# A convolution and two MLPs on one core: TensorE's instruction stream as one loop in place of seven passes written out

## The chip, the core and the metric

The kernel runs on one core of one Trainium2 chip. The core has five engines, each with an instruction queue of its own: PE (TensorE, matmuls), DVE (VectorE), ACT (ScalarE), POOL (GpSimd) and SP (SyncE, which here issues nearly all the DMAs). They meet only through semaphores. The metric is the time of one execution on the device, in microseconds (us). Before the change it is 1183.47 us, the median of 3 runs (1183.36 to 1183.52).

## The reference

The input x has 2 x 4096 rows of 192 numbers. Three things are done to it in turn: a causal filter over time with 7 softmax-weighted taps per head, and two MLPs from 192 to 2048 and back to 192.

```python
w = softmax(weight, axis=-1)                     # 8 heads, 7 taps
attn = sum over k of w[head, k] * x_pad[s + k]   # causal, zeros ahead of row 0
x1 = attn.reshape(8192, 192)

h = x1 @ moe_w_in                                # 192 -> 2048
x2 = np.maximum(0.01 * h, h) @ moe_w_out         # leaky, back to 192

h = x2 @ moe2_w_in
g = np.where(h >= 1, h, np.where(h <= -1, 0.0, (h + 1) ** 2 / 4))
out = g @ moe2_w_out
```

All of it is float32 in the reference.

## The kernel before

**Tiles and jobs.** The 8,192 rows are cut into 16 tiles of 512. Each tile is a leaky job (first MLP) and later a smooth job (second MLP), 32 jobs in all. A job takes the 2,048 hidden units in 16 chunks of 128. For a chunk, PE makes the hidden block (192 rows of weights against 512 columns of the tile, in high and low parts of the numbers, so that the product is as exact as float32), ACT and DVE apply the activation and split the result into a high part `g_hi` and a low part `g_lo`, and PE multiplies these by the second weights into two accumulators, `acc_edge` and `acc_main`.

**Matmuls in pairs.** Nearly every matmul uses 64 of the 128 rows of the array. `top_first` and `top_second` use the upper half, `bottom_first` and `bottom_second` the lower, and the code writes them in turn, so that one of either half runs at a time. One step of `two_chunks` writes 38 matmuls: 18 that open two chunks and finish the pair six chunks back (lines 338 to 348 and 430 to 442), then 20 in `second_half` (lines 401 to 414 and 360 to 374). A job has 8 such steps, 304 matmuls.

**Order.** Each engine's program is written by hand. The first two jobs fill the pipeline. Then come 7 passes (`PASSES`) of four jobs each, `loop_jobs(j)`: smooth, leaky, smooth, leaky. Then two last smooth jobs.
Of the kernel before, what the change touches and what calls it, by code (L numbers as in the profile page):

```python
# [34 lines left out]
def is_number(v, *numbers):  # L35

    return type(v) is int and v in numbers
# [7 lines left out]
def bass_conv_mlp_mlp(nc, x, weight, moe_w_in, moe_w_out, moe2_w_in, moe2_w_out, out):  # L45
# [24 lines left out]
    with ExitStack() as ctx:  # L70
# [112 lines left out]
        def leaky_job(n, a, t, b, prev, load=None, finish=None, at=4):  # L183
            return dict(n=n, a=a, at=at, layer=LEAKY, t=t, b=b, prev=prev, load=load, finish=finish)

        def smooth_job(n, a, t, b, prev, finish=None):
            return dict(n=n, a=a, layer=SMOOTH, t=t, b=b, prev=prev, load=None, finish=finish)

        first_jobs = [
            leaky_job(0, 0, 0, EVEN, None, load=(1, ODD, 0), finish=(1, ODD), at=1),  # L190
            leaky_job(1, 1, 1, ODD, (LEAKY, 0, EVEN), load=(2, EVEN, 1)),
        ]
        PASSES = (TILES - 2) // 2

        def loop_jobs(j):

            return [
                smooth_job(4 * j + 2, 0, 2 * j, EVEN, (LEAKY, 2 * j + 1, ODD), finish=(2 * j + 2, EVEN)),
                leaky_job(4 * j + 3, 1, 2 * j + 2, EVEN, (SMOOTH, 2 * j, EVEN),
                          load=(2 * j + 3, ODD, j + 1)),  # L200
                smooth_job(4 * j + 4, 0, 2 * j + 1, ODD, (LEAKY, 2 * j + 2, EVEN), finish=(2 * j + 3, ODD)),
                leaky_job(4 * j + 5, 1, 2 * j + 3, ODD, (SMOOTH, 2 * j + 1, ODD),
                          load=(2 * j + 4, EVEN, j + 2)),
            ]

        last_jobs = [
            smooth_job(2 * TILES - 2, 0, TILES - 2, EVEN, (LEAKY, TILES - 1, ODD)),
            smooth_job(2 * TILES - 1, 1, TILES - 1, ODD, (SMOOTH, TILES - 2, EVEN)),
        ]
        JOBS = 2 * TILES  # L210

        def all_jobs(engine, run):
            for job in first_jobs:
                run(job)
            with engine.Fori(0, PASSES) as j:
                for job in loop_jobs(j):
                    run(job)
            for job in last_jobs:
                run(job)
# [13 lines left out]
        def _(sp):  # L233
# [18 lines left out]
            def load_weights(piece):  # L252
                l, q = piece // PIECES, piece % PIECES
                s, _, _, rows, _ = piece_parts(piece)
                loaded = stage_loaded[piece % AHEAD]
                w = w_in_dram[l][:, q * PW:(q + 1) * PW]
                sp.dma_start(s[:, 0:PW], w[0:P]).then_inc(loaded, 16)
                for r in (0, EDGE):
                    sp.dma_start(s[r:r + EDGE, PW:2 * PW], w[P:D]).then_inc(loaded, 16)
                sp.dma_start(rows, w_out_dram[l][:, q * PC:(q + 1) * PC, :]).then_inc(loaded, 16)  # L260
# [60 lines left out]
        def _(pe):  # L321
# [155 lines left out]
            def opening(job):  # L477

                for i in range(5):
                    top_first(job, 0, i)
                for i in range(2):
                    top_first(job, 1, i)
                for i in range(2):
                    top_first(job, 1, i + 2)
                    bottom_first(job, 0, i)
                for i in range(2):
                    top_first(job, 2, i)
                    bottom_first(job, 0, i + 2)  # L490
                for i in range(3):
                    top_first(job, 2, i + 2)
                    bottom_first(job, 1, i)
                for i in range(2):
                    top_first(job, 3, i)
                    bottom_first(job, 1, i + 3)
                for i in range(2):
                    top_first(job, 3, i + 2)
                    bottom_first(job, 2, i)
                for i in range(2):  # L500
                    top_first(job, 4, i)
                    bottom_first(job, 2, i + 2)
                for i in range(3):
                    top_first(job, 4, i + 2)
                    bottom_first(job, 3, i)
                for i in range(2):
                    top_first(job, 5, i)
                    bottom_first(job, 3, i + 3)
                for i in range(2):
                    top_first(job, 5, i + 2)  # L510
                second_half(job, 4)

            def two_chunks(job, c):

                for i in range(5):
                    top_first(job, c, i)
                    bottom_second(job, c - 6, i)
                for i in range(4):  # L520
                    top_first(job, c + 1, i)
                    bottom_second(job, c - 6, i + 5)
                second_half(job, c)

            def run(job):
                opens = is_number(job["n"], 0)
                if opens:
                    opening(job)
                for c in range(6 if opens else 0, CHUNKS, 2):
                    two_chunks(job, c)  # L530
                if is_number(job["n"], 1):
                    pe.wait_ge(stage_used, 2 * PIECES)
# [8 lines left out]
            pe.wait_ge(warm_ready, 1)  # L541
            for _ in range(WARM):
                nc.tensor.matmul(acc_main[1][:], g[0][:, 0:P], g[0][:], start=True, stop=True)
            for job in first_jobs:
                run(job)
            for j in range(PASSES):
                for job in loop_jobs(j):
                    run(job)
            for job in last_jobs:
                run(job)  # L550
            for i in range(10):
                bottom_second(last_jobs[-1], CHUNKS - 6, i)
            for c in range(CHUNKS - 4, CHUNKS):
# [3 lines left out]
        def _(act):  # L557
# [46 lines left out]
            def top_smooth(prev):  # L604

                _, t, b = prev
                act.wait_ge(edge_step, 2 * t + 1)
                nc.scalar.copy(op_top[SMOOTH][b][EDGE:P, :], edge_sum[:]).then_inc(op2_top_ready, 1)
# [58 lines left out]
        def _(dve):  # L667
# [99 lines left out]
            def between_main(prev, a):  # L767

                _, t, b = prev
                dve.wait_ge(op2_hi_ready, t + 1)  # L770
                nc.vector.tensor_tensor(op_lo[SMOOTH][b][:], acc_main[a][:],
                                        op_hi[SMOOTH][b][:].bitcast(F32), ALU.subtract).then_inc(acc_taken, 1)
# [131 lines left out]
```

## Time and profile before

| | |
|---|---|
| Median of 3 runs | 1183.47 us |
| The profiled execution | 1183.36 us |
| Its span, first to last instruction | 1181.6 us |
| PE matmuls busy | 1155.8 us, 98% of the span |
| PE weight loads busy (they overlap the matmuls) | 924.5 us, 78% |
| DVE busy | 920.8 us, 78% |
| ACT busy | 793.2 us, 67% |
| POOL busy | 61.1 us, 5% |
| Granted TensorE clock, mean | 0.992 of full speed |

The profile is of one execution, and its times are read against that execution's 1183.36 us. Of PE, the profile has two kinds of rows: matmuls and weight loads as the array ran them, and on PE's queue (written PEldq) the semaphore, register and branch instructions as the queue executed them. The queue runs ahead of the array. Rows with ACTq, DVEq and SPq are of the other engines' queues. "q8 instruction" and "q14 instruction" are DMA queues that bring instructions, not data. In a strip of 40 slices, each digit is the busy share of a fortieth of the stretch in tenths, and serves here to place a packet in time. The clock is given as a share of 2.4 GHz: 1.00 is that, 0.50 is 1.2 GHz.

### The profile page before, as it was taken

The page shows a single profiled execution, that of the slowest core. Times are in us where ns is not written, and L with a number is a line of the kernel's source. Part 1 is how long each engine was busy: PE and PEld are TensorE (multiplying, and loading weights), DVE is VectorE, ACT ScalarE, POOL GpSimd, SP SyncE. Part 2 cuts the span into 40 slices and gives each one's busy share as a digit, 9 for nine tenths or more (in the row PEclk, how much of TensorE's full clock was granted, in tenths as well). Part 3 has the DMA queues.
Part 4 walks back from the last instruction along what each step waited for, and adds up shares of the span by engine and source line. Part 5 has one row for each costly group of instructions (what it writes and reads, how often), then busy time and mean ns, then how long its engine had stood idle before and what let it go on. Part 6 is the DMA issues. An engine that isn't in the chain of part 4 may idle for free.

```text
span 1181.6 us, 25758 instructions
## 1 busy us (share of the span) xinstructions
PE 1155.8 (98%) x9726; PEld 924.5 (78%) x9726; DVE 920.8 (78%) x1525; ACT 793.2 (67%) x1457; POOL 61.1 (5%) x73
## 2 busy tenths in 40 slices
PE   6889999999999999999999999999999999999998
PEld 3567888888888888888888888888888888888886
DVE  6988787777888778787777788777887777878665
ACT  3566757667585775757667585675857667586685
POOL 4762000000000000000000000000000000000000
PEclk8989999999999999999999999999999999999999
DMA  4330010010101001010010101001010010100001
GB/s 120 90 86 10 1 28 1 14 17 1 28 1 28 3 1 28 1 28 3 12 17 1 29 2 28 1 2 29 1 28 1 12 19 1 28 1 15 1 1 27
DMA packets 114468, 22.18 MB, mean 19 GB/s; under 512 B 106128, under 2 KB 114320, under 8 KB 114320
## 3 DMA queue, kind: packets, MB, share of 16 engines
q1 hardware_dynamic: 114304, 20.34, 9.3%
q8 instruction: 77, 1.26, 0.5%
q14 instruction: 71, 0.58, 0.2%
q10 hardware_dynamic: 16, 0.00, 0.0%
HBM read 14.02 MB, written 6.29 MB: 17 GB/s over the span
## 4 chain that ended last, share of the span: by engine, by line
PE 92%; DVE 5%; ACT 1%; issue 1%; SPq 0%; DMA 0%; DVEq 0%; ACTq 0%
PE hidden L348 14%; PE hidden L340 10%; PE acc_edge L404 10%; PE hidden L342 9%; PE acc_edge L401 9%; PE hidden L344 9%; PE acc_main L412 9%; PE acc_main L414 9%; PE acc_main L410 9%; DVE conv_main L691 1%; DVE g L748 1%; DVE conv_edge L703 1%; DVE g_lo L759 0%; ACT pre L577 0%; ACT g_hi L596 0%
## 5 line engine op out<-in xcount | busy, mean ns | idle before, releaser
L596 ACT CAST g_hi<-g 128x512 fp32r<-128x512 f32 x512 | 300.4, 619 | 300.2 <-PE acc_main L442 247.4
L759 DVE TENSOR_TENSOR g_lo<-g,g_hi 128x512 fp32r<-128x512 f32 x512 | 335.7, 690 | 120.7 <-ACT g_hi L596 116.0
L348 PE MATMUL hidden<-op_edge,w_edge 64*128 64x512 f32 x768 | 262.2, 395 | 1.6 <-DVE op_edge L736 1.6
L753 DVE SCALAR_TENSOR_TENSOR g<-hidden,pre 128x512 f32<-128x512 f32 x256 | 176.7, 690 | 105.6 <-ACT pre L584 102.6
L340 PE MATMUL hidden<-op_hi,w_main 64*128 64x512 f32 x512 | 203.5, 398 | 13.1 <-DVE op_lo L716 5.7
L360 PE MATMUL hidden<-op_hi,w_main 64*128 64x512 f32 x512 | 202.4, 395 | 0.0
L404 PE MATMUL acc_edge<-g_lo,w_out 64*128 64x512 f32 x508 | 200.8, 395 | 1.5 <-DVE g_lo L759 1.5
L342 PE MATMUL hidden<-op_lo,w_main 64*128 64x512 f32 x512 | 202.1, 395 | 0.0
L364 PE MATMUL hidden<-op_hi,w_main 64*128 64x512 f32 x512 | 202.0, 395 | 0.0
L344 PE MATMUL hidden<-op_hi,w_main 64*128 64x512 f32 x512 | 201.9, 394 | 0.0
L362 PE MATMUL hidden<-op_lo,w_main 64*128 64x512 f32 x512 | 201.4, 393 | 0.0
L367 PE MATMUL hidden<-op_edge,w_edge 64*128 64x512 f32 x512 | 201.2, 393 | 0.0
L430 PE MATMUL acc_edge<-g_hi,w_out 64*128 64x512 f32 x508 | 200.5, 395 | 0.0
L440 PE MATMUL acc_main<-g_hi,w_out 64*128 64x512 f32 x508 | 200.4, 394 | 0.0
L432 PE MATMUL acc_edge<-g_lo,w_out 64*128 64x512 f32 x508 | 199.9, 393 | 0.0
L442 PE MATMUL acc_main<-g_lo,w_out 64*128 64x512 f32 x508 | 199.8, 393 | 0.0
L401 PE MATMUL acc_edge<-g_hi,w_out 64*128 64x512 f32 x508 | 199.8, 393 | 0.0
L438 PE MATMUL acc_main<-g_hi,w_out 64*128 64x512 f32 x508 | 199.8, 393 | 0.0
L412 PE MATMUL acc_main<-g_hi,w_out 64*128 64x512 f32 x508 | 199.4, 392 | 0.0
L410 PE MATMUL acc_main<-g_hi,w_out 64*128 64x512 f32 x508 | 199.4, 392 | 0.0
L414 PE MATMUL acc_main<-g_lo,w_out 64*128 64x512 f32 x508 | 199.4, 392 | 0.0
L748 DVE SCALAR_TENSOR_TENSOR g<-pre 128x512 f32<-128x512 f32 x256 | 181.7, 715 | 22.5 <-ACT pre L577 22.3
(92 smaller groups left out, 2805.4 us busy)
## 6 DMA issues: line engine op xcount, KB each, us to landing
x_in<-in_x_dram SPq DMA_DIRECT2D x68, 64.0 KB, 2.3
out_dram<-y_main SPq DMA_DIRECT2D x64, 64.0 KB, 1.8
stage<-in_moe_w_out_dram SPq DMA_DIRECT2D x16, 192.0 KB, 2.7
x_in_edge<-in_x_dram SPq DMA_DIRECT2D x68, 32.0 KB, 2.0
stage<-in_moe_w_in_dram SPq DMA_DIRECT2D x16, 128.0 KB, 2.4
stage<-in_moe_w_in_dram SPq DMA_DIRECT2D x32, 64.0 KB, 2.4
out_dram<-y_edge SPq DMA_DIRECT2D x32, 64.0 KB, 1.8
taps_raw<-in_weight_dram ACTq DMA_DIRECT2D x1, 0.2 KB
```

Source lines behind the costliest of these rows:

```text
L340: nc.tensor.matmul(h[:], w_main[l][top, 0, cols], op_hi[l][b][top, :], start=True, stop=False)
L342: nc.tensor.matmul(h[:], w_main[l][top, 0, cols], op_lo[l][b][top, :], start=False, stop=False)
L344: nc.tensor.matmul(h[:], w_main[l][top, 1, cols], op_hi[l][b][top, :], start=False, stop=False)
L348: done = nc.tensor.matmul(h[:], w_edge[l][top, i - 3, cols], op_edge[l][b][top, :], start=False, stop=False)
L360: nc.tensor.matmul(h[:], w_main[l][bottom, 0, cols], op_hi[l][b][bottom, :], start=False, stop=False)
L401: nc.tensor.matmul(edge[:], w[:, P:2 * P], hi, start=k == 0, stop=False)
L404: done = nc.tensor.matmul(edge[:], w[:, P:2 * P], lo, start=False, stop=False)
L410: nc.tensor.matmul(main[:], w[:, 0:P], hi, start=k == 0, stop=False)
L412: nc.tensor.matmul(main[:], w[:, 2 * P:], hi, start=False, stop=False)
L414: done = nc.tensor.matmul(main[:], w[:, 0:P], lo, start=False, stop=False)
L596: nc.scalar.copy(g_hi[c % SLOTS][:], g[c % SLOTS][:]).then_inc(g_hi_ready, 1)
L759: nc.vector.tensor_tensor(g_lo[c % SLOTS][:], g[c % SLOTS][:], g_hi[c % SLOTS][:].bitcast(F32), ALU.subtract).then_inc(g_lo_ready, 1)
```

## The change

PE's program now calls `all_jobs` as ACT's and DVE's do. The helper is not changed:

```python
        def all_jobs(engine, run):
            for job in first_jobs:
                run(job)
            with engine.Fori(0, PASSES) as j:
                for job in loop_jobs(j):
                    run(job)
            for job in last_jobs:
                run(job)
```

```diff
@@ -541,13 +541,7 @@
             pe.wait_ge(warm_ready, 1)
             for _ in range(WARM):
                 nc.tensor.matmul(acc_main[1][:], g[0][:, 0:P], g[0][:], start=True, stop=True)
-            for job in first_jobs:
-                run(job)
-            for j in range(PASSES):
-                for job in loop_jobs(j):
-                    run(job)
-            for job in last_jobs:
-                run(job)
+            all_jobs(pe, run)
             for i in range(10):
                 bottom_second(last_jobs[-1], CHUNKS - 6, i)
```

In the built program PE's stream had 9,717 matmuls and 292 semaphore instructions in one piece. Now it has 567 matmuls ahead of the loop, 1,216 in its body and 638 behind it. The body also has 129 register operations, 16 fused register operations (shown as ISA), 30 semaphore instructions and the compare-and-branch; for the same four jobs the program before has 36 semaphore instructions and nothing else beside its matmuls. The order of the matmuls is the same. No other engine's program changes.

On PE, at the seam of two passes, the program before goes from the last matmuls of one leaky job straight to the first ones of the next smooth job:

```order
L412 MATMUL acc_main<-g_hi,w_out 128x512
L367 MATMUL hidden<-op_edge,w_edge 128x512
L414 MATMUL acc_main<-g_lo,w_out 128x512
L374 MATMUL hidden<-op_top,w_edge 128x512
L340 MATMUL hidden<-op_hi,w_main 128x512 [waits g_ready,op2_ready]
L430 MATMUL acc_edge<-g_hi,w_out 128x512 [waits edge_top_added]
L342 MATMUL hidden<-op_lo,w_main 128x512
```

On PE at the end of the loop's body the same matmuls are now followed by the loop's own instructions, L215, which is the line of `Fori`:

```order
L412 MATMUL acc_main<-g_hi,w_out 128x512
L367 MATMUL hidden<-op_edge,w_edge 128x512
L414 MATMUL acc_main<-g_lo,w_out 128x512
L374 MATMUL hidden<-op_top,w_edge 128x512
L215 REGISTER_ALU
L215 COMPARE_AND_BRANCH
```

The branch goes back to the head of the body, whose first rows on PE are these:

```order
L215 ISA
L339 ISA [waits op2_ready]
L340 MATMUL hidden<-op_hi,w_main 128x512 [waits g_ready]
L429 ISA
L430 MATMUL acc_edge<-g_hi,w_out 128x512 [waits edge_top_added]
L342 MATMUL hidden<-op_lo,w_main 128x512
L432 MATMUL acc_edge<-g_lo,w_out 128x512
L344 MATMUL hidden<-op_hi,w_main 128x512
L430 MATMUL acc_edge<-g_hi,w_out 128x512
```

The matmuls stand as before. Three fused register operations have come between them, and the wait on `op2_ready` has moved from a semaphore instruction to one of these.

## Rows read from the trace of the kernel before

**Rows 1.** The page: busy time with share and count; shares of the chain.

```profile
PE 1155.8 (98%) x9726; PEld 924.5 (78%) x9726; DVE 920.8 (78%) x1525; ACT 793.2 (67%) x1457; POOL 61.1 (5%) x73
...
PE 92%; DVE 5%; ACT 1%; issue 1%; SPq 0%; DMA 0%; DVEq 0%; ACTq 0%
```

**Rows 2.** Windows of one pass: stretch, busy us and count by engine, clock, DMA.

```profile
core 0: us, PE busy (x) PEld busy (x) DVE busy (x) ACT busy (x) POOL busy (x), PEclk, DMA share, GB/s
248.40:390.20 141.80, 141.80 (x1220) 114.44 (x1218) 111.43 (x188) 97.01 (x176) 0.00 (x0) 1.00 0.08 13
```

**Rows 3.** PE's timeline over two seams: start, us, instruction.

```profile
246.19 0.39 PE L414 MATMUL acc_main<-g_lo,w_out 64*128 64x512 f32 x1
...
246.43 0.40 PE L340 MATMUL hidden<-op_hi,w_main 64*128 64x512 f32 x1
...
388.29 0.40 PE L340 MATMUL hidden<-op_hi,w_main 64*128 64x512 f32 x1
```

**Rows 4.** The page, instruction queues: packets, MB, share of 16 engines.

```profile
q8 instruction: 77, 1.26, 0.5%
q14 instruction: 71, 0.58, 0.2%
```

**Rows 5.** L215 on ACT's queue, 246 to 256 us: count, ns, first and last start.

```profile
L215 ACTq ALU_OP  x1: 35/35/35, 249.0 to 249.0; - x1
L215 ACTq COMPARE_BRANCH  x1: 54/54/54, 249.0 to 249.0; - x1
L215 ACTq FUSED_REGOPS  x1: 68/68/68, 251.5 to 251.5; - x1
```

**Rows 6.** L215 on DVE's queue, the same stretch.

```profile
L215 DVEq COMPARE_BRANCH  x1: 63/63/63, 250.2 to 250.2; - x1
L215 DVEq FUSED_REGOPS  x1: 85/85/85, 253.2 to 253.2; - x1
```

**Rows 7.** L282 on SP's queue, 230 to 240 us.

```profile
L282 SPq COMPARE_BRANCH  x1: 59/59/59, 235.6 to 235.6; - x1
L282 SPq FUSED_REGOPS  x1: 50/50/50, 235.8 to 235.8; - x1
```

**Rows 8.** DMA in 40 slices of 249:251, then of 252.5:254.5, with instruction queues.

```profile
DMA  0000000000000000000400000000000000000000
...
q14 instruction: 1, 0.01, 1.2%
...
DMA  0000000000090000000000000600000000000000
...
q8 instruction: 1, 0.02, 3.7%
```

**Rows 9.** L400 on PE's queue, 414 to 416 us, and the matmul behind it.

```profile
L400 PEldq EVENT_SEMAPHORE  x1: 51/51/51, 415.2 to 415.2; - x1
...
416.99 0.39 PE L401 MATMUL acc_edge<-g_hi,w_out 64*128 64x512 f32 x1
```

**Rows 10.** L339 and L400 on PE's queue, 422 to 424.5 us.

```profile
L339 PEldq EVENT_SEMAPHORE  x1: 51/51/51, 422.6 to 422.6; - x1
...
L400 PEldq EVENT_SEMAPHORE  x1: 51/51/51, 424.1 to 424.1; - x1
```

**Rows 11.** L339 on PE's queue, 103 to 104 us, and its matmul.

```profile
L339 PEldq EVENT_SEMAPHORE  x1: 722/722/722, 103.3 to 103.3; - x1
...
104.41 0.39 PE L340 MATMUL hidden<-op_hi,w_main 64*128 64x512 f32 x1
```

**Rows 12.** L400 on PE's queue; DMA in 40 slices of 105.5:107.5.

```profile
L400 PEldq EVENT_SEMAPHORE  x1: 51/51/51, 105.4 to 105.4; - x1
...
DMA  0000000000000000000900000000000000000000
```

**Rows 13.** PE behind its long gap, and windows of two early stretches.

```profile
63.88 0.79 PE L340 MATMUL hidden<-op_hi,w_main 64*128 64x512 f32 x1 [4.09 <-DVE op_edge L736]
...
97.00:103.00 6.00, 4.44 (x32) 2.52 (x30) 6.00 (x10) 3.16 (x6) 1.28 (x2) 1.00 0.00 0
64.00:69.40 5.40, 5.40 (x26) 4.27 (x28) 4.11 (x5) 1.79 (x5) 4.17 (x4) 0.50 0.16 38
```
## The prediction

> **What bounds the kernel now.** I read the page first: PE is busy 98% of the span, and the chain of work that ended last lies on PE for 92% of it [rows 1]. Then the windows: in a pass of the loop over tiles PE is busy in all of 141.8 us, at clock 1.00 (2.4 GHz), while DVE works 111.4 and ACT 97.0 us of it [rows 2]. So what is put between two matmuls comes back in the time, and what is put on DVE or ACT does not, up to some 30 us a pass. Then PE's timeline over the seam of two passes: pairs of 64-row matmuls start every 0.233 us, with no step between the last L414 of one pass and the first L340 of the next, and that L340 comes again 141.86 us later [rows 3]. The seam is where the change puts a jump.
>
> Two things more have to be read. One is where PE's instructions come from. Queue q8 moved 77 packets, 1.26 MB; PE ran 9,726 matmuls and as many weight loads [rows 1, 4]. 1.26 MB over 19,452 is 65 bytes each (64, with the few semaphore instructions that the page does not count), so a packet of 16 KB brings 256 instructions. The other is what engines that already loop pay for their jump. ACT's compare-and-branch is at 249.0 us and its next instruction at 251.5 [rows 5]; DVE's are at 250.2 and 253.2 [rows 6]. SP, with 62 instructions in its body, goes on after 0.2 us [rows 7]. ACT's body has 312 instructions and DVE's 352, and q14 brings 0.58 MB / 71 = 8 KB, 128 instructions, at a time [rows 4]: their loop heads lie 2.4 and 2.8 blocks back, and are fetched again. On ACT the packet starts at 249.95 to 250.0, 0.9 us behind the branch, lasts 1.2% of 16 engines' 2 us, 0.38 us, and 1.15 us later the first instruction runs [rows 5, 8].
>
> **The change, part by part.** It removes no matmul. Seven passes written out become seven turns of one body: 1,216 matmuls, 1,216 weight loads, 129 register operations, 16 fused ones, 30 semaphore waits and one branch, 2,608 instructions, against 2,468 for a pass now. The body is 10.2 blocks of 256, and there are six jumps back.
>
> The 140 added instructions I cost at nothing. What hides them is the lead of PE's queue over its array. The semaphore instruction ahead of the L401 of 416.99 us ran at 415.2: the queue is 1.78 us, some 15 matmuls, ahead [rows 9]. Where its lead had been cut, it passed 18 matmuls with their loads (36 instructions and a wait) between 422.6 and 424.1 us, 41 ns each at most [rows 10]; the array needs 58 (0.233 us for four). So a pass has 2,468 x 17 ns = 42 us of room, and the new instructions want 140 x 35 to 68 ns (ACT's register operation and its fused one [rows 5]), 5 to 10 us. Without that cover they would cost 34 to 67 us in all; a gain is excluded, since nothing is taken from the array.
>
> The jump is the term that counts. Register add and branch take 0.08 us [rows 5]; branch to fetch 0.9; a packet of 16 KB in place of 8, which took 3.7% of 16 engines' 2 us, 1.2 us [rows 8]; landing to first instruction 1.15. That is 3.3 us between branch and body. (From below it is ACT's 2.4 us as it stands; from above 3.9, for DVE's slower restart and a packet that meets others.) From the end of a wait in the queue to the matmul behind it: the wait of L339 ended at 103.3 + 0.72 = 104.0 and its L340 started at 104.41 [rows 11], 0.4 us; with the two fused operations at the loop head, 0.5. Meanwhile the array eats the lead of 1.78 us. It idles 0.08 + 3.3 + 0.5 - 1.78 = **2.1 us** (1.2 to 2.8).
>
> The Trainium skill (Advanced Engine Details and Errata, Engine Queue Depths) gives TensorE a queue of 64. By it 32 matmuls would lie ahead, 3.7 us, and 0.2 us of the jump would show. The trace disagrees, with 1.78 us, and the trace decides.
>
> Then the second block. Now a q8 packet starts at 106.45 to 106.5 us; the L400 wait at 105.4 stands 37 instructions behind the first L340 of the passes, and at 41 to 58 ns apiece the queue passes some 20 more until then, so the packet starts about 57 instructions behind the place that becomes the loop head [rows 12]. On DVE the packet after the restart begins 0.6 us after it (253.2, then 253.75 to 253.8 [rows 6, 8]). If crossing into a block triggers the fetch with that lag, the boundary is 45 instructions behind the head (38 to 57). The stream ahead of the head does not change, so after a jump only 45 instructions are there: about 19 matmuls, which last the array until 0.5 + 9.5 x 0.233 = 2.7 us after the restart. The next block starts to come at 0.6, takes 1.2, and can run at 2.95; its first matmul starts 0.4 later, at 3.35. The array idles another **0.65 us** (0 to 1.0).
>
> Sum: 2.75 us a jump, six times, 16.5 us (7 to 23). The profiled execution took 1183.36 us, 0.1 less than the median of 1183.47: 1183.4 + 16.5 = 1199.9, so **1200**. Nothing gives it back, since the array has no later idle time to catch up in. DVE's and ACT's own refetches (2.5 to 3 us) come 3 to 4 us after PE's, when the array's late start has left them with less to do, so I add nothing for them. Entering and leaving the loop I put at nothing: that is reading straight on.
>
> The Trainium skill (Runtime: NRT & Kernel Launch, Instruction fetch mechanics) says that PE holds 2,048 instructions and that a taken branch out of what is held stalls for the fetch. By that rule too the head of 2,608 is gone; no run here shows the size.
>
> **The rivals.**
> *The clock falls too.* Behind the one long gap of PE in the run, 4.09 us up to 63.88, the clock was 0.50 (1.2 GHz) until 69.4: 26 matmuls in 5.4 us, where a pass does some 46 [rows 2, 13]. From 97 to 103 us PE was idle for 1.6 of 6 us, in pieces, and it stayed at 1.00 [rows 13]. My 2.1 us in one piece lies between. A fall costs 20 matmuls of 0.117 us, 2.3 us or a little more: 14 us at all six jumps, 1214; 7 at half of them, 1207.
> *The jump is free, and the time does not rise.* If PE keeps the head of its body, the jump costs what SP's does, 0.2 us, and a lead of 1.78 us swallows it: 1183.5. It decides from the point where PE keeps 10.2 blocks; ACT and DVE did not keep 2.4.
> *The lead is deeper than the semaphore instructions show.* If they wait for the queue to drain while matmuls go ahead of it freely, the lead at the branch may be twice as long: 3.88 - 3.56 = 0.32 us a jump, no second stall, 1185.5. The Trainium skill's queue of 64 would be this.
> *The queue becomes the bound.* PE's plain semaphore instruction takes 51 ns [rows 9], where ACT's register operation takes 35, so register work may be slower there too. To matter, the 140 must cost over 42 us a pass, 300 ns each. Then 34 us or more come on top of the jumps: 1234 and up.
>
> **How the numbers follow.** The forecast, 1200 with its own spread of 1190 to 1206: 0.64. Clock falls at some or all jumps: 0.18, 1203 to 1217. Free jump: 0.08. Deeper lead: 0.05. Queue bound: 0.05. The range for 8 in 10 is 1191 to 1217; it leaves out the free jump, the deeper lead, the queue bound and a few per cent of the forecast's edges. A measurement of this kernel tells 0.2% (2.4 us) from no change. Within that lie the free jump and most of the deeper lead, 0.11; faster has no mechanism, 0.01; slower 0.88.
>
> **What would show it.** In the new profile: six gaps of PE at the first L340 behind a pass, put down to no other engine, 1.2 to 2.8 us each; a shorter one some 19 matmuls on; passes of about 144.6 us; elsewhere 0.233 us a pair. On PE's queue the branch some 3.3 us ahead of the next instruction. q8 at 77 packets or a few more. PEclk at 1.00 behind the gaps. It is wrong if passes stay at 141.9 us (head kept, or a deeper lead), if pairs are wider than 0.233 us all along a pass (queue bound), or if the clock reads 0.5 behind a jump.

## The result and the profile after

The changed kernel takes 1211.24 us, the median of 4 runs (1207.78 to 1212.90), against 1183.47. The ratio is 1.0231, 95% interval 1.0206 to 1.0255: 27.8 us slower. The forecast was 1200, range 1191 to 1217. The profiled execution took 1208.51 us, its span 1206.7.

The page after, its busy line, the strip of the clock and PE's instruction queue:

```profile
PE 1166.5 (97%) x9726; PEld 1050.9 (87%) x9726; DVE 919.0 (76%) x1525; ACT 793.5 (66%) x1457; POOL 62.2 (5%) x73
...
PEclk8999999999999999999999999999999999999999
...
q8 instruction: 94, 1.54, 0.6%
...
L340 PE MATMUL hidden<-op_hi,w_main 64*128 64x512 f32 x512 | 205.4, 401 | 25.4 <-issue 12.4 <-DVE g L742 7.3 <-DVE op_edge L730 4.1
```

PE is still the bound (97%, where it had 98% [rows 1]). Its L340 now has 25.4 us of idle time ahead of it, half of that put down to "issue", to no engine: before, its whole idle time there was 13.1 us. q8 brought 94 packets instead of 77 [rows 4].

PE's timeline over the first jump back (start, us, instruction, idle time before and what ended it), where before nothing lay between L414 and L340 [rows 3]:

```profile
243.73 0.39 PE L374 MATMUL hidden<-op_top,w_edge 64*128 64x512 f32 x1
...
246.59 0.79 PE L340 MATMUL hidden<-op_hi,w_main 64*128 64x512 f32 x1 [2.47 <-issue]
246.73 0.79 PE L430 MATMUL acc_edge<-g_hi,w_out 64*128 64x512 f32 x1
247.18 0.62 PE L342 MATMUL hidden<-op_lo,w_main 64*128 64x512 f32 x1
```

From L374 to L340 it is 2.86 us instead of 0.23: a gap of 2.63. And the pairs behind it start 0.43 to 0.59 us apart, not 0.233: the array is slow. What PE's queue did meanwhile, over the whole run and at this jump (count, ns as least/median/most, first and last start):

```profile
L215 PEldq COMPARE_BRANCH  x7: 76/3979/5133, 242.3 to 1121.2; - x7
...
L215 PEldq COMPARE_BRANCH  x1: 3981/3981/3981, 242.3 to 242.3; - x1
L215 PEldq FUSED_REGOPS  x1: 50/50/50, 246.4 to 246.4; - x1
```

The branch row holds the whole wait here: it takes 3.98 us, and the loop head follows at 246.4. At every one of the six jumps L340 starts 0.28 to 0.29 us behind the end of this row, also where the page puts the idle time down to DVE's g: so it is the branch that held it, not DVE. The row with 76 ns is the seventh, which is not taken. DMA in 40 slices of 0.2 us, at the first jump and at the third:

```profile
DMA  0000000000000001003000000000000000300000
...
q8 instruction: 2, 0.03, 1.9%
...
DMA  0000000516000000000000000000000003000000
...
q8 instruction: 3, 0.05, 4.0%
```

At the first jump a q8 packet starts at 243.6 to 243.8, 1.3 us behind the branch of 242.3, and the next at 246.8 to 247.0, 0.5 us behind the restart (the digit at 243.0 to 243.2 is one of q14). At the third, two q8 packets start 0.4 us apart, in the slices of 535.4 and 535.8 (digits 5 and 6), 0.7 and 1.1 us behind the branch, and are under way together; the three of that stretch take 4.0% x 16 x 8 us / 3 = 1.7 us each on average, those of the first jump 1.9% x 16 x 8 / 2 = 1.2.

A window behind the first jump (stretch, its length, busy us and count of PE, PEld, DVE, ACT and POOL, clock, DMA share, GB/s), and PE's second gap behind the fifth:

```profile
246.50:249.90 3.40, 3.31 (x16) 3.31 (x18) 0.00 (x0) 0.00 (x0) 0.00 (x0) 0.50 0.02 5
...
831.67 0.49 PE L340 MATMUL hidden<-op_hi,w_main 64*128 64x512 f32 x1 [2.14 <-DVE g L742]
...
835.05 0.50 PE L401 MATMUL acc_edge<-g_hi,w_out 64*128 64x512 f32 x1 [0.90 <-issue]
```

For 3.4 us the clock is 0.50 (1.2 GHz): 16 matmuls, where a pass does 29 in that time [rows 2]. At 835.05, 18 matmuls behind the restart, the array stands idle a second time.

**The account.** Taking each time from the last L414 before a jump (at the first jump it starts with the L374 shown) to the L340 behind it, less 0.233, the six gaps are 2.63, 2.69, 3.98, 2.07, 2.35 and 3.95 us, 17.7 in all. The clock was at 0.50 for 3.4 us behind five of them, 1.5 to 1.7 us each, 8.2 in all. The second stall is 1.2 us at the fifth jump and 0.3 at the sixth. Together 27.4. The seven passes last 27.6 us more than seven times 141.87 [rows 3]. That is close to the median's 27.8, though only one execution was profiled. That one was only 25.15 us slower because its first pass began at 101.95 us, not 104.41; in the profiles of the twelve experiments below it began between 102.5 and 105.5, so I put this down to the execution, not to the jump.

### The profile page after: what moved, and what is told of

The parts are those of the page before. It is cut to its first block, busy times and chain, and to the rows that moved or that the text cites. A ratio compares the mean times of both kernels' runs of the same rounds, so it can differ in the third digit from the quotient of the medians.

```text
span 1206.7 us, 26739 instructions
## 1 busy us (share of the span) xinstructions
PE 1166.5 (97%) x9726; PEld 1050.9 (87%) x9726; DVE 919.0 (76%) x1525; ACT 793.5 (66%) x1457; POOL 62.2 (5%) x73
## 4 chain that ended last, share of the span: by engine, by line
PE 91%; DVE 5%; ACT 2%; issue 1%; SPq 0%; DMA 0%; DVEq 0%; ACTq 0%
PE hidden L348 9%; PE hidden L340 6%; PE acc_edge L401 6%; PE acc_edge L404 6%; PE hidden L342 6%; PE acc_main L410 6%; PE hidden L344 6%; PE acc_main L412 6%; PE acc_main L414 6%; PE acc_main L440 4%; PE acc_main L438 4%; PE acc_edge L432 4%; PE acc_edge L430 4%; PE acc_main L442 4%; PE hidden L360 3%; PE hidden L362 3%
## 5 line engine op out<-in xcount | busy, mean ns | idle before, releaser
L340 PE MATMUL hidden<-op_hi,w_main 64*128 64x512 f32 x512 | 205.4, 401 | 25.4 <-issue 12.4
L414 PE MATMUL acc_main<-g_lo,w_out 64*128 64x512 f32 x508 | 199.2, 392 | 0.0
```

Source lines behind the costliest of these rows:

```text
L340: nc.tensor.matmul(h[:], w_main[l][top, 0, cols], op_hi[l][b][top, :], start=True, stop=False)
L414: done = nc.tensor.matmul(main[:], w[:, 0:P], lo, start=False, stop=False)
```

## The experiments

The edits are shown against the kernel before, whose lines they replace, with long lines broken. Gaps and clock are those of each run's one profiled execution.

**One turn: the register work without a jump.**

```diff
-            for j in range(PASSES):
-                for job in loop_jobs(j):
-                    run(job)
+            with pe.Fori(0, 1) as j:
+                for turn in range(PASSES):
+                    for job in loop_jobs(j + turn):
+                        run(job)
```

> The seven passes written out again, inside a loop of one turn, so that every wait still depends on a register and every register operation is there, but no jump is taken. Theory A: passes of 141.9 us, no gap, 1181 to 1185 us. Theory B (register work costs it): 1207 to 1213 us, or at least a pair of matmuls wider than 0.233 us in places.

Measured 1183.34 us, ratio 0.9999 (0.9989 to 1.0009). PE's timeline at the seam of its first two passes:

```profile
245.56 0.39 PE L374 MATMUL hidden<-op_top,w_edge 64*128 64x512 f32 x1
245.79 0.40 PE L340 MATMUL hidden<-op_hi,w_main 64*128 64x512 f32 x1
```

From pair to pair 0.233 us, and every pass 141.87 (the first 142.0, as before). Register operations and register waits on PE cost nothing here. Theory B is out.

**Two jumps instead of six.**

```diff
-            for j in range(PASSES):
-                for job in loop_jobs(j):
-                    run(job)
+            for job in loop_jobs(0):
+                run(job)
+            with pe.Fori(0, 3) as j:
+                for half in (1, 2):
+                    for job in loop_jobs(2 * j + half):
+                        run(job)
```

> One pass written out with constants, then a loop of three turns with two passes in its body: six of seven passes keep their register work, but two jumps are taken, not six. Theory A: two gaps of 2.0 to 4.0 us, each with a stretch of 3.4 us at clock 0.5 or not, a third of the changed kernel's 27 us: 1189 to 1195 us. Theory B (register work): 6/7 of it, 1203 to 1211 us.

Measured 1190.78 us, ratio 1.0059 (1.0041 to 1.0077): 7.4 us, 3.7 a jump. Both gaps are 2.3 us, and the clock fell behind both. The cost goes with the number of jumps. It is a little under a third of 27.8: neither jump had a gap of 4 us, and the two unprofiled executions near 1189.5 us have a mean clock of 0.993, like the kernel before, where the other two have 0.990, so the clock may not have fallen in them.

**The place of the loop head.** Two runs move it within its fetch block of 256 instructions; `head_slot` is its place there.

```diff
-            for j in range(PASSES):
+            with nc.Fori(0, PASSES, engines=bass.OrderedEngineSet([mybir.EngineType.PE]),
+                         head_slot={mybir.EngineType.PE: 0}) as j:      # and with 220
```

> The changed kernel, with the loop head placed at the first instruction of a fetch block. Then 256 instructions are there after a jump, not some 45, and the body's end lies 48 instructions behind a block's start, not 2 or 3. Theory A with its two additions (a second stall where the next block is late; gaps of 4.0 us where the block behind the body is being fetched when the branch asks for its target): six gaps of 2.0 to 2.7 us, no second stall, none of 4 us, three fetches of q8 around no jump in flight together; time 1202 to 1208 us, some 4 us under the changed kernel. If the head's place does not matter: 1207 to 1213 us with one or two gaps of 4 us.

Measured 1203.57 us, ratio 1.0164 (1.0146 to 1.0183). The six gaps are 2.0 to 2.5 us, there is no second stall, and the clock fell behind four. As the theory had it, though the gain on the changed kernel is 7.7 us and not 4.

> The changed kernel with the head at slot 220, so that the branch stands some 11 instructions behind its block's start and the fetch of the block behind the body is under way at every jump. Theory of the collision (the two gaps of 4 us of the changed kernel came from that fetch standing in the target's way): gaps of 3.3 to 4.1 us at all or nearly all six jumps, two q8 packets within 1 us at each, time 1211 to 1220 us. If the 4 us came from something else (other DMA traffic): gaps mostly 2.0 to 2.7 us and 1205 to 1213 us.

Measured 1209.43 us, ratio 1.0212 (1.0195 to 1.0229), under the 1211 to 1220 of the theory. Branch row over the run (eight here: the first, at 100.9 us, leads into the loop, and the last is not taken), and DMA around the first jump (slices of 0.2 us):

```profile
L546 PEldq COMPARE_BRANCH  x8: 76/4196/5003, 100.9 to 1124.0; - x8
...
DMA  0000000070600000000000000000000003000000
...
q8 instruction: 3, 0.05, 4.0%
...
248.30 0.79 PE L340 MATMUL hidden<-op_hi,w_main 64*128 64x512 f32 x1 [3.64 <-issue]
```

Four jumps, not six, have two q8 packets side by side, and these four have gaps of 3.5 to 3.8 us; the two with a single packet have 2.3 and 2.4. So the pairing of two packets with a long gap holds at every jump, but my claim that this slot brings it at every jump missed: whether the packet of the block behind is already asked for when the branch comes still depends on something finer. In the changed kernel the same was true of two jumps in six. With slot 0 it was true of none: at two jumps a packet started 0.6 and 1.7 us ahead of the branch and was over before the target's began, and at the other four none started in the 6 us before.

**The hint, alone and with a place.** The loop can put an instruction at its head that announces the branch at its end, so that the target's block may be fetched early.

```diff
-            for j in range(PASSES):
+            with nc.Fori(0, PASSES, engines=bass.OrderedEngineSet([mybir.EngineType.PE]),
+                         hint_back_edge=True) as j:
```

> The changed kernel, with a prefetch hint for the branch at the head of PE's loop body, so that the head's block can be asked for ahead of the jump. All register operations and all six jumps stay. Theory A (the jump waits for its target's instructions): the gaps of 2.0 to 4.0 us at the first L340 of a pass go, passes are near 141.9 us, the clock does not fall, time 1182 to 1188 us. Theory B (register operations, register waits or the branch as such cost the time): as the changed kernel, 1207 to 1213 us.

Measured 1205.74 us, ratio 1.0185 (1.0167 to 1.0204). That is just under theory B's range and far from A's; but the one-turn kernel rules B out, so the hint must have failed in its work. The trace says so: the hint ran at each turn, yet the branch rows stay long and the q8 packet starts 1 us behind the branch (245.9; slices of 0.2 us from 244).

```profile
L546 PEldq BRANCH_PREFETCH_HINT  x7: 36/40/45, 104.0 to 979.3; - x7
...
L546 PEldq COMPARE_BRANCH  x7: 88/3652/3756, 245.9 to 1121.2; - x7
...
DMA  0000000000000140000000000000000030000000
```

The gaps are 2.1 to 2.6 us and none is 4. Since, by the prediction's count of 45 instructions to the first block start, the branch stands 2 or 3 instructions behind its block's start, I supposed that the hint acts when that block is entered, which here is too late. At the second and the sixth jump, the two behind which the clock did not fall, the array stands idle again 17 matmuls on:

```profile
399.24 0.38 PE L440 MATMUL acc_main<-g_hi,w_out 64*128 64x512 f32 x1 [0.79 <-issue]
```

The next run adds a place to the hint; its edit is against the run with the hint alone.

```diff
-                         hint_back_edge=True) as j:
+                         hint_back_edge=True, head_slot={mybir.EngineType.PE: 40}) as j:
```

> The prefetch hint as in the first experiment, and the loop head placed at slot 40 of a fetch block, so that the branch stands 89 instructions (some 5 us) behind the start of its block. With the hint alone no fetch had come ahead of the branch, and there the branch stood 2 or 3 instructions behind a block's start. Theory C: the hint takes effect where the block of the branch is entered, and turns the fetch made there to the branch's target. Then one q8 fetch lands well ahead of each branch, the gaps at the first L340 of a pass go, the clock stays, and the time is 1181 to 1186 us. Theory D (the hint does nothing on this engine): as with the head at slot 0, 1201 to 1206 us, gaps of 2.0 to 2.5 us.

Measured 1182.13 us, ratio 0.9991 (0.9982 to 1.0001). Branch rows (again with one that leads into the loop), DMA from 240 us on, and the seam:

```profile
L546 PEldq COMPARE_BRANCH  x8: 80/434/475, 103.4 to 1096.5; - x8
...
DMA  4532715403000000000000000000001030000000
...
q8 instruction: 2, 0.03, 1.6%
...
246.71 0.39 PE L374 MATMUL hidden<-op_top,w_edge 64*128 64x512 f32 x1
246.94 0.40 PE L340 MATMUL hidden<-op_hi,w_main 64*128 64x512 f32 x1
```

A taken branch now takes 0.43 to 0.48 us, which the lead covers; L374 to L340 is 0.233 us again, every pass 141.87 (the first 142.0), and the clock does not fall. The fetch is now ahead of the branch of 245.3: the stretch holds two q8 packets, one from 241.8 on (the digit 3 behind the load of x, which fills 240.0 to 241.6), 3.5 us ahead of the branch, and the next block's from 246.4 on. Theory C fits: with its target at hand, a jump of this loop costs nothing. Slot 40 without the hint was not run, so what the place does by itself is open; slots 0 and 220 without a hint waited 3.4 to 5.0 us at each jump.

> The loop with the hint and its head at slot 40, again, in five rounds, to see whether it is the same as the kernel written out or faster by the tenth of a per cent that three rounds left open. Same: 1182 to 1184 us, interval across 1. Faster: an interval below 1.

Measured 1181.87 us, ratio 0.999 (0.9981 to 0.9999). That is 0.1% under the kernel before, with an interval that just stays under 1. Its passes are as long as before; in its profiled execution the first one begins at 102.61 us, where before it was 104.41, and the medians differ by 1.5 us. Why it begins earlier there I do not know; in the earlier run of the same kernel it began at 104.94.

**How large a body is free.** Behind the kernel's work, six idle loops on PE.

```diff
+            pe.wait_ge(y_edge_ready, TILES)
+            for size in (100, 480, 860, 900, 1000, 1100):
+                with nc.Fori(0, 3, engines=bass.OrderedEngineSet([mybir.EngineType.PE]),
+                             head_slot={mybir.EngineType.PE: 0}):
+                    for _ in range(size):
+                        nc.tensor.matmul(hidden[0][:, 0:P], w_main[1][:, 0, 0:P], w_main[1][:, 1, 0:P], ...)
```

> The kernel before, with PE's program followed by six idle loops of three turns each, of 100, 480, 860, 900, 1000 and 1100 matmuls of 128 columns (about 200, 960, 1720, 1800, 2000 and 2200 instructions), heads at the start of a block. Their results go to a bank that nobody reads; the time is not to be compared. It asks from what size on a jump waits for its target. If PE keeps as little as ACT and DVE (under 2.4 blocks of theirs): only the first loop jumps without a gap. If it keeps eight blocks of 256 but fetches one ahead: 100, 480 and 860 jump free and 900 and over show gaps of 3 to 4 us. If all eight serve: 1000 is free too and only 1100 pays.

It ran for 4022.64 us, which says nothing. The branch rows of a taken jump in the loops of 860, 900 and 1,100 matmuls, and a window inside the loop of 860:

```profile
L557 PEldq COMPARE_BRANCH  x1: 208/208/208, 1913.1 to 1913.1; - x1
...
L557 PEldq COMPARE_BRANCH  x1: 3531/3531/3531, 2288.6 to 2288.6; - x1
...
L557 PEldq COMPARE_BRANCH  x1: 3697/3697/3697, 3547.3 to 3547.3; - x1
...
1700.00:2000.00 300.00, 300.00 (x1408) 300.00 (x1408) 0.00 (x0) 0.00 (x0) 0.00 (x0) 0.50 0.00 0
```

Up to 1,720 instructions the target is still there, and a taken branch takes 0.21 us. From 1,800 on, 7.04 blocks with the loop's own instructions, it is fetched; there a q8 packet also starts 1.5 us ahead of each of the two jumps back, which the loop of 860 does not have. So PE keeps much more than ACT and DVE, yet not what the body of 10.2 blocks needs. The expectation of gaps failed: the array is late by 0.06 us at most. Its matmuls are 0.213 us apart there, one at a time and not in pairs, at a clock of 0.50 throughout, and at the jumps of 1,000 and 1,100 where it is late, the last of 18 matmuls behind the branch starts 3.7 us after it. In the changed kernel 11 to 14 start behind the branch and are done in 1.5 to 1.65 us. So what lies ahead is nearer to a number of matmuls than to a time. Why the clock stayed at 0.50 in these loops was not tried.

**Idle time without a jump.** Does the clock fall because of the jump or because of the gap? Here the passes are written out and PE's queue is held by waits that are long satisfied. In the built program one semaphore instruction carries two of them, so that 164 waits make 82 ("An instruction carries one wait", said of the kernel before, is not so of these).

```diff
             for j in range(PASSES):
+                for k in range(164 if j else 0):      # then 116, 76, 56
+                    pe.wait_ge((weights_ready, stage_used)[k % 2], 1)
```

> The kernel before, all passes written out and no jump, with 82 semaphore instructions (51 ns each, all long satisfied) ahead of passes 2 to 7 on PE. They hold PE's queue for 4.2 us, as long as the jump of the changed kernel does, and take 4.2 - 1.8 of lead = 2.4 us from the array. If the fall of the clock comes of the idle time alone: gaps of 2.2 to 2.6 us, the clock at 0.50 for 3.4 us behind most of the six, passes of 144.3 us with 1.7 more where it fell, 1204 to 1209 us in all. If the fall needs the jump or its fetch: no fall, 1197 to 1200 us.

> The same with 58 semaphore instructions, 3.0 us, of which the lead takes 1.8: gaps of 1.1 to 1.4 us. If the lead is worth the same 1.8 us here, 6 x 1.2 = 7 us on top, and if gaps of this size leave the clock alone as those of the start did (1.0 us), 1190 to 1192 us; if the clock falls behind them too, 1196 to 1201 us.

Measured 1238.3 us (ratio 1.0464, 1.0448 to 1.048) and 1222.72 (1.0332, 1.0316 to 1.0348). Both missed, and by one fault of mine: 82 instructions held the queue for 8.7 us and 58 for 6.1, since one, with its two waits, starts 106 ns behind the other though its row says 51. The gaps were 7.1 and 4.5 to 4.8 us. At all 24 seams of this run and of the three others of its kind, 14 matmuls start behind the first semaphore instruction, and the last of them is done 1.8 us behind it; the first L340 then starts some 0.3 us behind the end of the hold. The clock fell behind all twelve gaps. Then with the right count:

> The two runs before held the queue longer than meant, since each semaphore instruction took 106 ns from one to the next, not the 51 of its row; their gaps were 7.1 and 4.5 us. So here 38 of them, 4.0 us, no jump: 4.0 + 0.2 - 1.8 = gaps of 2.3 to 2.5 us, those of the changed kernel. If the clock falls for the idle time alone: at most of the six gaps, 1.7 us each, and 1183.4 + 14.4 + 5 to 10 = 1203 to 1208 us. If it needs the jump: 1197 to 1199 us, no fall.

> 28 semaphore instructions, 3.0 us: gaps of 1.3 to 1.5 us. If gaps of that size leave the clock alone, as those of 1.0 us at the start do: 6 x 1.4 = 8 us on top, 1191 to 1193 us, PEclk 1.00 behind them. If it falls behind some: up to 10 us more, 1193 to 1202 us.

Measured 1204.05 us (1.0176, 1.0159 to 1.0193) and 1192.01 (1.0073, 1.0056 to 1.0089). PE at the first seam of the shorter and a window behind it, then windows of the longer behind two of its seams (columns as above):

```profile
247.71 0.47 PE L340 MATMUL hidden<-op_hi,w_main 64*128 64x512 f32 x1 [1.16 <-DVE g L750]
...
247.70:252.00 4.30, 4.29 (x37) 3.97 (x39) 1.23 (x3) 1.14 (x2) 0.00 (x0) 1.00 0.02 6
...
249.10:252.50 3.40, 3.40 (x30) 3.13 (x32) 0.12 (x1) 0.77 (x2) 0.00 (x0) 1.00 0.00 0
393.90:397.30 3.40, 3.40 (x20) 3.01 (x18) 0.00 (x0) 0.00 (x0) 0.00 (x0) 0.52 0.00 0
```

With gaps of 1.3 to 1.4 us the clock stays at 1.00 at all six; with gaps of 2.4 us, and no jump at all, it fell behind three of six, for 3.4 us each; with gaps of 4.5 us or more always. So the fall needs no jump: it goes with the idle time. At the jumps, too, it came behind all six gaps of 3.5 to 4 us and behind some of those of 2.0 to 2.7. What decides within that band was not tried.

## Why the prediction was right, and where it was short

By its own signs the forecast itself did not come true: the clock read 0.5 behind jumps, which was named as a sign that it is wrong, and 1211.24 lies above its spread of 1190 to 1206 and in that of the rival with the clock (1203 to 1217). The range held because it took in that rival. The change did what was forecast for the reason that was forecast, the wait of PE's queue for the target's instructions; the sizes of its terms were off.

- **What bounds the kernel; DVE and ACT have room.** Right. What PE's array lost came back whole: 27.4 us found in gaps, slow stretches and second stalls, 27.6 in the passes.
- **The 140 added instructions at nothing.** Right: one turn with all of them measures 0.9999, and every pass but the first (142.0, as before) is 141.87 us.
- **The jump refetches its target, 3.3 us from branch to body; the array idles 2.1 us (1.2 to 2.8).** Right in kind. Four of six jumps had gaps of 2.07 to 2.69 us, 2.4 on average. There the fetch began 1.0 to 1.6 us behind the branch, where I took ACT's 0.9; the packet took 0.9 to 1.2, where I took 1.2; from its landing to the loop head it was 1.4 to 1.5, where I took 1.15. That makes 3.35 to 3.98 us, not 3.3. From the head to L340 it was 0.3, not 0.5. Two of six had 4.0 us, above the bound: I had seen that the second block comes late, and not that the block behind the body may be on its way when the branch asks for its own, so that two packets share the queue: they took 1.7 to 2.2 us each, and the branch 5.05 and 5.13. That boundary could have been worked out from the prediction's own estimate: 45 instructions from the head to the first block start leave the end of a body of 2,608 at 2,608 - 45 - 10 x 256 = 3 behind a start. The step that failed is the upper bound of the gap, 2.8 us, where 3.98 was measured.
- **A lead of 1.78 us, about 15 matmuls.** Right. The runs with a held queue give 1.8 us and 14 matmuls beside the pair that is running; from the branch of a jump it was 1.5 to 1.65 us and 11 to 14 matmuls. The Trainium skill (Advanced Engine Details and Errata, Engine Queue Depths) gives TensorE a queue of 64. By that figure, an estimate, each gap would have been some 1.9 us shorter (32 matmuls of 0.117 us in place of 1.8 us); no run bears that out.
- **The second block late by 0.65 us at each jump.** Mis-sized. It showed fully once (1.2 us) and partly once (0.3). At the other four the array ran at half clock behind the gap, and its 18 matmuls then lasted long enough to hide it. The run with the hint alone agrees: its two second stalls, of about 1 us, stand behind the two jumps at which the clock did not fall. With the head at slot 0 none showed, so the mechanism stands. I summed 3.9 us; it was 1.5.
- **The clock.** It was a rival at 0.18, with 2.3 us a fall; it should have been part of the forecast. It fell behind five of six jumps, and each fall cost 1.6 us, since the slow stretch was 3.4 us, where [rows 13] had shown 5.4 behind the restart. That is 8.2 us, the largest part of what 1200 was short by. That an idle array is enough for it, without a jump, is shown by the runs that hold the queue.
- **The sum.** 16.5 us were forecast: 12.6 of first gaps, 3.9 of second. Measured: 17.7, 1.5, and 8.2 of clock. The errors, +5.1, -2.4 and +8.2, leave the time 11 us over the forecast and inside the range. That the second term was too large made up for half of what the first lacked, which is luck.
- **The free jump** is refuted for this body and right for bodies of up to 1,720 instructions. The Trainium skill (Runtime: NRT & Kernel Launch, Instruction fetch mechanics) gives 2,048; here 1,800 was already too many, and the measurement decides. A block fetched ahead of need would explain it, and the packet ahead of the jumps of that loop fits, though no run separates that.
- **The branch itself.** It took 0.08 us untaken, 0.21 taken with the target held in the idle loops, 0.43 to 0.48 with the hint at slot 40, 3.3 to 5.1 when the target had to be fetched behind it. The Trainium skill (Advanced Engine Details and Errata, Control Flow Timing) has about 0.11 us for a compare-and-branch; no row here shows that value, and the measurements decide.

## What to carry to other kernels

An engine that is the bound can be put in a loop at no cost if the jump's target is at hand each time: keep the body small enough, or announce the branch and place it well behind the start of its block (89 instructions here; no other place was tried with the hint, except the 2 or 3 that did not serve), and read the branch's own row on the queue to see whether that worked. Without it, price a jump as the wait less what the queue has ahead, and then ask what the gap does to the clock. A rival that the rows cannot rule out and that repeats at every jump belongs in the sum with its chance.

## What the runs showed of the hardware that was not expected

- PE's taken branch took 208 ns with a body of 1,720 instructions and 3,531 ns with one of 1,800.
- A hint at the loop head changed nothing with the branch 2 or 3 instructions behind its block's start (branch 3.65 us at the median), and removed the wait with the branch 89 behind (0.43 us).
- Two instruction packets side by side took 1.5 to 2.4 us each, where one alone took 0.9 to 1.7 (median 1.1); every gap of 3.5 to 4 us in the changed kernel and at slot 220, six in all, had such a pair, and no other gap had.
- Semaphore instructions with two waits each follow each other on PE's queue at 106 ns, though their rows show 51. Whether those with one wait do was not run.
- In the six idle loops, PE at work on matmuls of 128 columns with no pause over 0.06 us and the other engines done, the clock stayed at 0.50, from 1178 us to the end of that run at 4021.
- Behind an idle array without a jump the clock stayed at 2.4 GHz for gaps of 1.3 to 1.4 us (6 of 6), fell for gaps of 2.4 us in 3 of 6, and for gaps of 4.5 us and more in 12 of 12. At jumps it fell for gaps of 3.5 to 4 us in 6 of 6.
